# Attention heads taken in pairs with full-precision value products, and a rewritten order of the MLP behind them

## The chip, the cores and the metric

One core of a Trainium2 chip runs the whole program. The metric is the device time of one execution in microseconds. Five engines matter: TensorE (PE in the profile; its weight loads are PEld), VectorE (DVE), ScalarE (ACT), GpSimd (POOL), and SyncE (SP), which here only issues DMAs.

## The reference, cut to what matters

```python
q, k, v: (4, 8, 576, 64) float32      # batch, heads, sequence, head_dim
def _attn_ref(q, k, v):
    q_rot, k_rot = rotate(q), rotate(k)            # rotary position, halves of 32
    scores = matmul(q_rot, k_rot.T) / sqrt(64)
    attn = exp(scores - max(scores)); attn = attn / (sum(attn) + 1e-9)
    return matmul(attn, v)
x = attn_out as (2304, 512)
def _moe_ref(x, w_in, w_out, g_ln):                # 512 -> 1024 -> 512
    h = x @ w_in
    solu = h * softmax(h)
    ln = (solu - mean) / sqrt(var + 1e-6) * g_ln
    return ln @ w_out
```

## The kernel before, in words

The attention works head by head, 32 heads, and holds the scores transposed: keys on partitions, queries along the row. A sequence of 576 is cut into five tiles of keys (four of 128, one of 64), and every product is done in two halves of 288 queries. TensorE is fed in fp32r, a reduced form of float32; precision is kept by splitting a number into a high part and a rest. The scores of a tile are two products, `KK` by `QQ` and `KB` by `QB` (L760): the rests stand in the lower 64 partitions, and `QB` also carries the negated row maximum. That maximum comes from products of its own (L748), reduced by VectorE (L526). Queries and keys arrive untransposed, so TensorE transposes them through PSUM (L725) and ScalarE copies them out (L349).

The exponentials of a tile (`p_full`, ScalarE, L369) are split: a high copy `p_hi` by ScalarE or VectorE (L343, L533), and a rest `p_lo` by GpSimd (L259; the 64-row tile by VectorE, L539). V is split too (L332, L268). Then `weigh` (L778) multiplies three ways per tile: `v_hi` by `p_hi`, `v_hi` by `p_lo`, `v_lo` by `p_hi`, and two ways for the tile of 64, whose rest is stacked below it. The columns of ones in V give the row sums. VectorE and GpSimd share the rotation (L496, L510; L252). VectorE also inverts the sums with two transposes (L546, L551), and GpSimd multiplies by the inverse (L264).

The order on each engine is written out by hand in its `step` function, and semaphores tie the engines together. There is one PSUM slot for scores: scores of a tile wait for the exponentials of the one before. The loops over heads and tiles are hardware loops (`Fori`).

The MLP works on 18 tiles of 128 tokens. For each tile TensorE does eight transposes of the normalized rows (L803), 24 products with `w_in` of a later tile (`up`, L788) and 24 with `w_out` (`down`, L815), all with 512 columns: three products for each true one. VectorE splits x (L572, L574), takes the maximum (L579), multiplies (L591), computes statistics (L596) and the normalized rows (L614), and subtracts the high part (L584). ScalarE does the exponentials (L391), the high part (L396) and the output (L402).

Of the kernel before, what the change touches and what calls it, by code (L numbers as in the profile page):

```python
# [11 lines left out]
AX_X = mybir.AxisListType.X  # L12
AX_XY = mybir.AxisListType.XY

P = 128
B, H, S, D = 4, 8, 576, 64
HEADS = B * H
PAIRS = HEADS // 2
NT = -(-S // P)
TAIL = S - (NT - 1) * P  # L20
SP_ = NT * P
HALF = S // 2
TOK = B * S
# [10 lines left out]

START = 1


def attention_then_mlp(nc: bass.Bass, qk_d, v_d, rope_d, w_d, gain_d, out_d):

    ctx = ExitStack()

    def sb(stack, name, shape, dt=F32):
        return stack.enter_context(nc.sbuf_tensor(name, shape, dt))

    def sem(stack, name):
        return stack.enter_context(nc.semaphore(name))

    with ctx:
        xT = sb(ctx, "xT", [P, KC * TOK])
        w_hi = sb(ctx, "w_hi", [P, NW * 512], F32R)
        w_lo = sb(ctx, "w_lo", [P, NW * 512], F32R)
        ident = sb(ctx, "ident", [P, P])
        ps = ctx.enter_context(nc.psum_tensor("ps", [P, 8, 512], F32))
        qk = [sb(ctx, f"qk{a}", [P, 2, NT, D]) for a in range(2)]
        v = [sb(ctx, f"v{a}", [P, NT, D]) for a in range(2)]
        rope = sb(ctx, "rope", [P, 2, NT, D])
        rot = sb(ctx, "rot", [P, 2, NT, D])  # L60
        crossed = sb(ctx, "crossed", [P, 2, NT, D])
        k_splits = sb(ctx, "k_splits", [P, 2, NT, 2 * D])
        q_twices = sb(ctx, "q_twices", [P, 2, NT, 2, D])
        q_rests = sb(ctx, "q_rests", [P, 2, NT, 2 * D])
        k_split = [k_splits[:, a, :, :] for a in range(2)]
        q_twice = [q_twices[:, a, :, :, :] for a in range(2)]
        q_rest = [q_rests[:, a, :, :] for a in range(2)]
        KK = [sb(ctx, f"KK{a}", [P, SP_], F32R) for a in range(2)]
        KB = [sb(ctx, f"KB{a}", [P, SP_], F32R) for a in range(2)]
        QQ = [sb(ctx, f"QQ{a}", [P, SP_], F32R) for a in range(2)]  # L70
        QB = [sb(ctx, f"QB{a}", [P, SP_], F32R) for a in range(2)]
        v_hi = [sb(ctx, f"v_hi{a}", [P, NT, P], F32R) for a in range(2)]
        v_lo = [sb(ctx, f"v_lo{a}", [P, NT, P], F32R) for a in range(2)]
        p_full = [sb(ctx, f"p_full{i}", [P, S]) for i in range(3)]
        p_parts = sb(ctx, "p_parts", [P, 2 * NT - 1, S], F32R)
        p_hi = [p_parts[:, j, :] for j in range(NT)]
        p_lo = [p_parts[:, NT + j, :] for j in range(NT - 1)]
        o_num = sb(ctx, "o_num", [P, S])
        o_sum = sb(ctx, "o_sum", [P, S])
        sum_cols = sb(ctx, "sum_cols", [P, S])  # L80
        inv_cols = sb(ctx, "inv_cols", [P, S // 32])
        inv = sb(ctx, "inv", [P, S])
        eps = sb(ctx, "eps", [P, 1])
        w_raw = sb(ctx, "w_raw", [P, 512])
        gain = sb(ctx, "gain", [P, NW])

        prep = [ps[:, 0:2, :], ps[:, 2:4, :]]
        prep_flat = [ps[:, 2 * i:2 * i + 2, :].rearrange("p a c -> p (a c)") for i in range(2)]
        scores = ps[:, 4:6, :]
        o_ps = ps[:, 6:8, :]  # L90

        qk_loaded = [sem(ctx, f"qk_loaded{a}") for a in range(2)]
        v_loaded = [sem(ctx, f"v_loaded{a}") for a in range(2)]
        rope_loaded = sem(ctx, "rope_loaded")
        gain_loaded = sem(ctx, "gain_loaded")
        w_loaded = sem(ctx, "w_loaded")
        w_hi_done = sem(ctx, "w_hi_done")
        w_lo_done = sem(ctx, "w_lo_done")
        cos_done = sem(ctx, "cos_done")
        sin_done = sem(ctx, "sin_done")  # L100
        sin_part_done = sem(ctx, "sin_part_done")
        rot_done = sem(ctx, "rot_done")
        k_hi_done = sem(ctx, "k_hi_done")
        k_lo_done = sem(ctx, "k_lo_done")
        q_hi_done = sem(ctx, "q_hi_done")
        q_lo_done = sem(ctx, "q_lo_done")
        kb_done = sem(ctx, "kb_done")
        v_hi_done = sem(ctx, "v_hi_done")
        v_lo_done = sem(ctx, "v_lo_done")
        prep_filled = [sem(ctx, f"prep_filled{i}") for i in range(2)]  # L110
        prep_free = [sem(ctx, f"prep_free{i}") for i in range(2)]
        scores_ready = sem(ctx, "scores_ready")
        exp_done = sem(ctx, "exp_done")
        p_hi_done = [sem(ctx, f"p_hi_done{j}") for j in range(NT)]
        p_lo_done = sem(ctx, "p_lo_done")
        p_tail_done = sem(ctx, "p_tail_done")
        pv_done = sem(ctx, "pv_done")
        o_taken = sem(ctx, "o_taken")
        inv_done = sem(ctx, "inv_done")
        x_done = sem(ctx, "x_done")  # L120
        ident_zero = sem(ctx, "ident_zero")
        pool_const = sem(ctx, "pool_const")
        dve_const = sem(ctx, "dve_const")
        POOL_CONST, DVE_CONST = 10, 8

        x_hi = [KK[0][:, 0:KC * P].rearrange("p (c t) -> p c t", c=KC),
# [829 lines left out]
```

## Time and profile before

| | us |
|---|---|
| median of 3 runs | 669.5 |
| lowest, highest run | 669.39, 672.09 |
| span of the profiled execution | 671.9 |
| PE, PEld busy | 569.8, 506.1 |
| DVE busy | 570.5 |
| ACT, POOL busy | 356.4, 354.2 |

The time of the profiled execution itself is not recorded apart from the three runs; its span lies between the median and the highest of them, 0.2 us below the highest. The span goes from the first instruction to the last. In a matmul row the duration counts the whole path through the array, so two rows overlap; the distance from one start to the next is what a matmul costs.

### The profile page before, as it was taken

To read this page: it belongs to the slowest core of one execution; us is meant where nothing else is said; L and a number is where in the kernel's file an instruction comes from. 1 tells how busy PE (TensorE), PEld (TensorE's weight loads), DVE (VectorE), ACT (ScalarE), POOL (GpSimd) and SP (SyncE) were. 2 spreads that over 40 slices of the span, in tenths; PEclk is the share of its full clock that TensorE was granted. 3 is DMA by queue.
4 is the path that set the end of the run, shared out by engine and by line. 5 is a ranking of instruction groups with operands and counts; after the bars stand their busy time and mean duration, and the time that the engine had idled before them with its cause. 6 is when DMAs were issued, how large, how long until landed. Compare 5 with 4: busy or idle time off the path is not lost.

```text
span 671.9 us, 11250 instructions
## 1 busy us (share of the span) xinstructions
PE 569.8 (85%) x3400; PEld 506.1 (75%) x3400; DVE 570.5 (85%) x756; ACT 356.4 (53%) x586; POOL 354.2 (53%) x273
## 2 busy tenths in 40 slices
PE   7878767887687877877878778899999999999986
PEld 7767757777677776776778767887888888888865
DVE  8899999999999999999999999897766757566560
ACT  3877668576686766766867667651212122121211
POOL 5769688786887967868769687641000000000000
PEclk9999999798998989989889898899999999999998
DMA  4111211112101121121111210000000000000000
GB/s 129 44 47 31 74 45 29 45 29 74 45 29 45 34 70 45 29 68 40 40 45 29 74 45 10 16 1 18 16 16 31 16 31 16 30 17 16 31 17 31
DMA packets 14411, 25.12 MB, mean 37 GB/s; under 512 B 1728, under 2 KB 5824, under 8 KB 14400
## 3 DMA queue, kind: packets, MB, share of 16 engines
q1 hardware_dynamic: 14400, 24.98, 12.2%
q8 instruction: 6, 0.10, 0.1%
q14 instruction: 5, 0.04, 0.0%
HBM read 20.26 MB, written 4.72 MB: 37 GB/s over the span
## 4 chain that ended last, share of the span: by engine, by line
PE 37%; DVE 36%; issue 21%; DVEq 2%; ACT 2%; POOL 1%; DMA 1%; SPq 0%; ACTq 0%; POOLq 0%
PE ps L815 15%; PE ps L788 14%; DVE q_rests L526 10%; DVE p_parts L533 6%; DVE rot L496 5%; DVE KB L562 4%; DVE w_hi L557 3%; DVE k_splits L515 2%; PE ps L803 2%; PE ps L778 2%; PE ps L760 2%; DVE rot L510 2%; PE ps L748 1%; DVE sum_cols L546 1%; PE ps L725 1%
## 5 line engine op out<-in xcount | busy, mean ns | idle before, releaser
L259 POOL TENSOR_TENSOR p_parts<-p_full,p_parts 128x576 fp32r<-128x576 f32 x128 | 201.5, 1578 | 87.8 <-ACT p_parts L343 48.7
L369 ACT ACTIVATE p_full<-ps 128x576 f32<-128x576 f32 (+1 forms) x160 | 103.9, 650 | 81.9 <-DVE p_parts L539 70.7
L760 PE MATMUL ps<-QQ,KK 128*128 128x288 f32 x320 | 82.3, 340 | 58.1 <-ACT p_full L369 58.1
L526 DVE TENSOR_REDUCE q_rests<-ps 128x1 fp32r<-128x576 f32 x160 | 114.3, 745 | 4.5 <-PE ps L748 4.4
L314 POOL TENSOR_TENSOR r<-r,expo 128x1 f32<-128x1 f32 x17 | 11.9, 698 | 185.3 <-DVE r L607 185.3
L748 PE MATMUL ps<-KK,QQ 128*128 128x288 f32 x320 | 82.0, 343 | 28.9 <-DVE q_rests L526 27.8
L778 PE MATMUL ps<-p_parts,v_hi 128*128 128x288 f32 x576 | 105.1, 301 | 0.0
L760 PEld LDWEIGHTS ps<-QQ,KK 128*128 128x128 f32 x320 | 51.3, 200 | 67.9 <-ACT p_full L369 66.4
L815 PE MATMUL ps<-w_hi,p_parts 128*128 128x512 f32 x288 | 94.3, 399 | 4.9 <-DVE p_parts L584 4.9
L778 PEld LDWEIGHTS ps<-p_parts,v_hi 128*128 128x128 f32 x576 | 89.2, 197 | 0.1
L748 PEld LDWEIGHTS ps<-KK,QQ 128*128 128x128 f32 x320 | 57.1, 214 | 40.8 <-DVE q_rests L526 39.3
L252 POOL TENSOR_TENSOR crossed<-qk,rope 128x320 f32<-128x320 f32 x63 | 78.1, 1258 | 1.4 <-DVE rot L510 1.4
L402 ACT ACTIVATE qk<-ps 128x512 f32<-128x512 f32 x18 | 10.8, 598 | 114.7 <-PE ps L815 114.7
L760 PE MATMUL ps<-QB,KB 128*128 128x288 f32 x320 | 71.5, 307 | 0.0
L778 PE MATMUL ps<-p_parts,v_lo 128*128 128x288 f32 x320 | 70.1, 301 | 0.0
L815 PEld LDWEIGHTS ps<-w_hi,p_parts 128*128 128x128 f32 x288 | 55.6, 193 | 18.5 <-issue 5.3
L343 ACT ACTIVATE p_parts<-p_full 128x576 fp32r<-128x576 f32 x96 | 65.4, 682 | 2.1
L579 DVE TENSOR_REDUCE neg_max<-ps 128x1 f32<-128x1024 f32 x18 | 22.0, 1224 | 52.0 <-PE ps L788 52.0
L815 PE MATMUL ps<-w_lo,p_parts 128*128 128x512 f32 x144 | 57.5, 399 | 0.0
L760 PEld LDWEIGHTS ps<-QB,KB 128*128 128x128 f32 x320 | 54.4, 199 | 0.0
L778 PEld LDWEIGHTS ps<-p_parts,v_lo 128*128 128x128 f32 x320 | 52.7, 193 | 0.0
L533 DVE CAST p_parts<-p_full 128x576 fp32r<-128x576 f32 x64 | 48.3, 754 | 2.2 <-ACT p_full L369 2.2
(86 smaller groups left out, 1145.4 us busy)
## 6 DMA issues: line engine op xcount, KB each, us to landing
qk<-qk_in SPq DMA_DIRECT2D x32, 320.0 KB, 3.2
v<-v_in SPq DMA_DIRECT2D x32, 160.0 KB, 2.3
out<-qk SPq DMA_DIRECT2D x18, 256.0 KB, 2.0
w_raw<-w_in SPq DMA_DIRECT2D x16, 256.0 KB, 2.6
rope<-rope_in SPq DMA_DIRECT2D x1, 320.0 KB, 3.5
gain<-gain_in SPq DMA_DIRECT2D x1, 8.0 KB, 4.2
```

Source lines behind the costliest of these rows:

```text
L252: ins = nc.gpsimd.tensor_tensor(crossed[:, :, :, to], qk[a][:, :, :, of], rope[:, 1:2, :, to].broadcast_to([P, 2, NT, 32]), ALU.mult)
L259: nc.gpsimd.tensor_tensor(p_lo[j][:, :], p_full[j % 3][:, :], p_hi[j][:, :], ALU.subtract).then_inc(p_lo_done, 1)
L343: nc.scalar.activation(p_hi[j][0:rows, :], p_full[j % 3][0:rows, :], ACT.Copy)\
L369: nc.scalar.activation(p_full[j % 3][0:rows, :].rearrange("p (b c) -> p b c", b=2), scores[0:rows, :, 0:HALF], ACT.Exp, scale=SCALE).then_ ...
L496: nc.vector.tensor_tensor(rot[:, :, :, :].rearrange("p s t d -> p s (t d)"), qk[a][:, :, :, :].rearrange("p s t d -> p s (t d)"), rope[:, ...
L526: nc.vector.tensor_reduce(q_rest[a][:, j, D:D + 1].bitcast(F32R), prep[slot][:, :, 0:HALF], AX_XY, ALU.max, negate=True).then_inc(prep_fre ...
L533: nc.vector.tensor_copy(p_hi[j][0:rows, :], p_full[j % 3][0:rows, :]).then_inc(p_hi_done[j], 1)
L748: ins = nc.tensor.matmul(prep[slot][:, half, 0:HALF], QQ[a][:, j * P:(j + 1) * P], KK[a][:, half * HALF:(half + 1) * HALF], start=True, st ...
L760: ins = nc.tensor.matmul(scores[:, half, 0:HALF], left[a][:, j * P:(j + 1) * P], right[a][:, half * HALF:(half + 1) * HALF], start=(k == 0 ...
L778: ins = nc.tensor.matmul(o_ps[:, half, 0:HALF], left[a][:, j, :], right[j][:, half * HALF:(half + 1) * HALF], start=(j == 0 and k == 0), s ...
L788: ins = nc.tensor.matmul(h_ps[a][:, half, :], left[a][:, c, :], right[:, col:col + 512], start=(c == 0 and k == 0), stop=(c == KC - 1 and ...
L815: ins = nc.tensor.matmul(y_ps[a], left[a][:, c * P:(c + 1) * P], right[:, col:col + 512], start=(k == 0), stop=(k == 3 * FC - 1))
```

## The change

The attention takes two heads at a time (16 pairs), and everything is written out without hardware loops.

- The host hands over q and k transposed, with a second copy whose halves are exchanged. So no transposes on TensorE: the rotation is one product with the cosines, one with the sines (both GpSimd, 128x1152), and one sum (VectorE, 128x1152).
- ScalarE writes the high parts straight into the stacks `QK` (`high`, `second_queries`) and copies keys into `KB` (`copy_keys`); VectorE writes the rests (`low_keys`, `low_queries`).
- The two 64-row tails of a pair share one tile: 9 steps a pair in place of 10.
- `weigh` multiplies V by the exponentials once, both in plain float32 (`V`, `p_main`, `p_tail` are no longer fp32r). No splits of P or V remain.
- The row maxima go through a 32x32 transpose and ten short DMAs into a row of `KB`. The row sums go by DMA into 9 columns (`sc`), ScalarE adds EPS, VectorE takes the reciprocal, and two DMAs through DRAM spread it over the partitions (`inv`).
- GpSimd divides the pair before last only after VectorE's rotation sum of the pair in hand.
- In the MLP the transposes stand between the `down` products, and `up` of the last tile stands before `down` of tile 14 instead of after it.

```diff
-                    parts = ((v_hi, p_hi), (v_hi, p_lo), (v_lo, p_hi))
-                else:
-                    pe.wait_ge(p_tail_done, START + h + 1)
-                    parts = ((v_hi, p_hi), (v_lo, p_hi))
-                for k, (left, right) in enumerate(parts):
-                    for half in range(2):
-                        ins = nc.tensor.matmul(o_ps[:, half, 0:HALF], left[a][:, j, :],
...
+                    p, v = p_main[(8 * n + 4 * a + j) % 3], V[c][:, a, 1 + j, :]
+                for half in range(2):
+                    ins = nc.tensor.matmul(o_ps[a][:, half, 0:HALF], v, p[:, half * HALF:(half + 1) * HALF],
+                                           start=(k in (0, 5)), stop=(k in (4, 9)))
+                ins.then_inc(pv_done, 1)
...
+            for n in range(PAIRS):
+                for s in range(STEPS):
+                    score(n, s)
+                    for i in maxima(n, s)[:1]:
+                        row_scores(n + 1, i)
...
+                    if s == 0:
+                        if n >= 1:
+                            weigh(n - 1, 9)
+                    elif s <= BOTH:
+                        weigh(n, s - 1)
+                    else:
+                        if s == BOTH + 1:
+                            weigh(n, 4)
+                        weigh(n, s)
...
+                if n + 2 < PAIRS:
+                    pool.wait_ge(low_q_done[1], n + 2)
+                    pool.wait_ge(w_lo_done, n - 1)
+                    pool.wait_ge(x_loaded[n % 2], uses(n + 2) * 16 - (0 if n % 2 else 32))
+                    times_cos(n + 2)
+                    times_sin(n + 2)
+                    pool.wait_ge(rot_done, n + 3)
+                if n >= 2:
+                    divide(n - 2)
...
+            def add_eps(m):
+                c = m % 2
+                act.wait_ge(sums_set[c], uses(m) * 32)
+                nc.scalar.activation(sc[c][:, :], sc[c][:, :], ACT.Copy, bias=EPS).then_inc(eps_done, 1)
...
+            for t in range(TILES):
+                if t + 3 == TILES - 1:
+                    for i in range(UPS):
+                        up(t + 3, i)
+                first = 16 if t == 0 else 4 if t + 3 < TILES else 0
+                for i in range(DOWNS):
+                    down(t, i)
+                    if t + 1 < TILES and first <= i < first + FC:
+                        transpose_ln(t + 1, i - first)
+                if t + 3 < TILES - 1:
+                    for i in range(UPS):
+                        up(t + 3, i)
```

TensorE in the middle of the attention, before; L725 are transposes, L760 scores, L748 products for the maxima, L778 the product with V:

```order
L725 MATMUL ps<-ident,k_splits 128x128 x5
L725 MATMUL ps<-ident,q_twices 128x128 x5
L757 ISA
L760 MATMUL ps<-QQ,KK 128x288 x2
L760 MATMUL ps<-QB,KB 128x288 x2
L771 ISA
L778 MATMUL ps<-p_parts,v_hi 128x288 x4
L778 MATMUL ps<-p_parts,v_lo 128x288 x2
L745 REGISTER_ALU
L748 MATMUL ps<-KK,QQ 128x288 x2
```

And now, steps 4 and 5 of a pair; L769 are scores, L742 the maxima, L791 the product with V:

```order
L769 MATMUL ps<-QK 128x288 x2
L769 MATMUL ps<-KB 128x288 x2
L769 MATMUL ps<-QK 128x288 x2
L769 MATMUL ps<-KB 128x288 x2
L742 MATMUL ps<-QK 128x288 x4
L791 MATMUL ps<-p_main,V 128x288 x2
L769 MATMUL ps<-QK 128x288 x2
L769 MATMUL ps<-KB 128x288 x2
L742 MATMUL ps<-QK 128x288 x2
L791 MATMUL ps<-p_tail,V 128x288 x4
```

The transposes are gone, and six products with V per tile are now two.

GpSimd in the middle of the attention, before (one head; L252 rotation, L259 rests of P, L268 rest of V, L264 division):

```order
L252 TENSOR_TENSOR crossed<-qk,rope 128x10x32 x2
L257 REGISTER_ALU
L258 ISA
L259 TENSOR_TENSOR p_parts<-p_full,p_parts 128x576
...
L268 TENSOR_TENSOR v_lo<-v,v_hi 128x5x64
...
L264 TENSOR_TENSOR xT<-o_num,inv 128x576
```

And now, a whole pair (L302 and L307 are the two products of the rotation, the rest the division):

```order
L302 TENSOR_TENSOR X<-X,rope 128x1152
L307 TENSOR_TENSOR X<-X,rope 128x1152
L315 TENSOR_TENSOR xT<-oe,inv 64x576
L317 TENSOR_TENSOR xT<-oe,inv 64x512
L320 TENSOR_TENSOR xT<-oe,inv 64x64
```

The eight rests of P and two of V per pair have gone; the whole of the rotation's products has come in.

## Rows read from the trace of the kernel before

**Rows 1.** Busy time by stretch: span, then PE, PEld, DVE, ACT, POOL busy (instructions), clock, DMA.
```profile
281.00:310.00 29.00, 22.71 (x154) 21.17 (x155) 28.68 (x34) 20.78 (x36) 22.71 (x17) 0.94 0.16 43
657.85:671.90 14.05, 8.36 (x33) 6.35 (x31) 1.22 (x1) 2.22 (x3) 0.00 (x0) 0.88 0.10 37
```
**Rows 2.** Who waited for whom in the attention, 49 to 440 us: total, times, longest.
```profile
PE ps L760 <- ACT p_full L369: 53.5, 29, 3.1
```
**Rows 3.** Groups by line and shape: busy us, mean ns | idle before.
```profile
L259 POOL TENSOR_TENSOR p_parts<-p_full,p_parts 128x576 fp32r<-128x576 f32 x128 | 201.5, 1578 | 87.8 <-ACT p_parts L343 48.7 <-DVE p_parts L533 38.9
L526 DVE TENSOR_REDUCE q_rests<-ps 128x1 fp32r<-128x576 f32 x160 | 114.3, 745 | 4.5 <-PE ps L748 4.4
L778 PE MATMUL ps<-p_parts,v_hi 128*128 128x288 f32 x576 | 105.1, 301 | 0.0
L778 PEld LDWEIGHTS ps<-p_parts,v_hi 128*128 128x128 f32 x576 | 89.2, 197 | 0.1
L369 ACT ACTIVATE p_full<-ps 128x576 f32<-128x576 f32 x128 | 83.3, 651 | 81.3 <-DVE p_parts L539 70.7 <-PE ps L760 9.1
L252 POOL TENSOR_TENSOR crossed<-qk,rope 128x320 f32<-128x320 f32 x63 | 78.1, 1258 | 1.4 <-DVE rot L510 1.4
L325 ACT ACTIVATE q_twices<-rot 128x640 fp32r<-128x640 f32 x32 | 23.2, 725 | 0.0
```
**Rows 4.** TensorE in order of time, in the attention: start, duration, group.
```profile
300.20 0.71 PE L725 MATMUL ps<-ident,q_twices 128*128 128x128 f32 x5
300.67 0.52 PE L760 MATMUL ps<-QQ,KK 128*128 128x288 f32 x2
301.02 0.43 PE L760 MATMUL ps<-QB,KB 128*128 128x288 f32 x2
301.29 0.68 PE L778 MATMUL ps<-p_parts,v_hi 128*128 128x288 f32 x4
301.81 0.43 PE L778 MATMUL ps<-p_parts,v_lo 128*128 128x288 f32 x2
```
**Rows 5.** VectorE and GpSimd in order of time, with and without each other.
```profile
6.63 0.83 DVE L510 TENSOR_TENSOR rot<-rot,crossed 128x640 f32<-128x640 f32 x1
301.49 1.85 POOL L264 TENSOR_TENSOR xT<-o_num,inv 128x576 f32 x1 [0.70 <-DVE inv L551]
302.06 1.88 DVE L539 TENSOR_TENSOR p_parts<-p_full,p_parts 64x576 fp32r<-64x576 f32 x1
318.28 0.75 DVE L539 TENSOR_TENSOR p_parts<-p_full,p_parts 64x576 fp32r<-64x576 f32 x1
320.65 1.42 POOL L259 TENSOR_TENSOR p_parts<-p_full,p_parts 128x576 fp32r<-128x576 f32 x1 [2.75 <-ACT p_parts L343]
```
**Rows 6.** Busy time in the fourth microsecond; the last number is GB/s.
```profile
3.00:4.00 1.00, 1.00 (x7) 1.00 (x6) 0.68 (x3) 0.00 (x0) 0.87 (x3) 1.00 1.01 397
```
**Rows 7.** DMA issues on the page: KB each, us to landing.
```profile
v<-v_in SPq DMA_DIRECT2D x32, 160.0 KB, 2.3
```
**Rows 8.** TensorE from the end of the attention into the MLP.
```profile
451.17 0.40 PE L788 MATMUL ps<-w_hi,KB 128*128 128x512 f32 x1
...
457.96 1.09 PE L803 MATMUL ps<-ident,q_rests 128*128 128x128 f32 x8 [1.17 <-DVE q_rests L614]
...
481.85 1.03 PE L803 MATMUL ps<-ident,q_rests 128*128 128x128 f32 x8
...
493.62 1.04 PE L803 MATMUL ps<-ident,q_rests 128*128 128x128 f32 x8
```
**Rows 9.** TensorE at the end of the MLP.
```profile
650.68 0.47 PE L815 MATMUL ps<-w_hi,p_parts 128*128 128x512 f32 x1 [2.46 <-DVE p_parts L584]
...
657.85 1.04 PE L803 MATMUL ps<-ident,q_rests 128*128 128x128 f32 x8
...
661.35 0.47 PE L815 MATMUL ps<-w_hi,p_parts 128*128 128x512 f32 x1 [2.46 <-DVE p_parts L584]
...
668.28 0.39 PE L815 MATMUL ps<-w_hi,p_parts 128*128 128x512 f32 x1
```

More of the change, by code:

```diff
@@ L65, in attention_then_mlp @@
[L65 to L72, printed above, removed]
@@ L82, in attention_then_mlp @@
[L82 to L94, printed above, removed]
@@ L178, in constants @@
[L178 to L188 removed]
+        x_hi_done = sem("x_hi_done")
@@ new lines, in attention_then_mlp, with x_of, uses, own @@
+        y_ready = sem("y_ready")
+        y_taken = sem("y_taken")
+        stored = [sem(f"stored{a}") for a in range(2)]
+        const_done = sem("const_done")
+        def x_of(m):
+            return xT[:, PAIRS - 4:PAIRS, :] if m == 2 else X[m % 2][:, :, :]
+        def uses(n):
+            return n // 2 + 1
+        def own(a):
+            return slice(a * D, a * D + D)
+        def other(a):
+            return slice((1 - a) * D, (1 - a) * D + D)
+        def last_pair(t):
+            return ((t + 1) * P - 1) // S * HP + HP - 1
@@ new lines, in row_part, with rows_of_a @@
+            def row_part(m, group, row, at, first, count, done):
+                n = count * TURN
+                sp.dma_start(KB[m % 2][row:row + 1, 1, at:at + n].bitcast(F32)
+                             .rearrange("o (p f) -> o p f", f=TURN),
+                             nm_row[group][first:first + (count - 1) * TURN + 1:TURN, :]).then_inc(done, 16)
+            def rows_of_a(m):
+                done = rows_early[m % 2]
+                sp.wait_ge(turned[0], m + 1)
+                for j in range(1 if m == 0 else BOTH):
+                    row_part(m, 0, D, main_col(0, j), j, 4, done)
+                row_part(m, 0, D, MAIN, BOTH, 2, done)
+                row_part(m, 0, 0, S + TAIL, D + BOTH, 2, done)
@@ L473, in _ @@
[L473 to L486 removed]
+                if t >= 2:
+                    act.wait_ge(stored[t % 2], t // 2 * 16)
@@ new lines, in _ @@
+            for n in range(1, PAIRS - 1):
+                for s in range(STEPS):
+                    for i in maxima(n, s):
+                        row_max(n + 1, i)
+                    if s == 0:
+                        low_keys(n + 1, 1)
+                        if n >= 2:
+                            invert(n - 2)
+                    if s == 1:
+                        low_queries(n + 1, 1)
+                    if s == 2 and n >= 2:
+                        w_low(n - 2)
+                    if s == 5 and n + 2 < PAIRS:
+                        add(n + 2)
+                    if s == 7 and n + 2 < PAIRS:
+                        low_keys(n + 2, 0)
+                    if s == 8 and n + 2 < PAIRS:
+                        low_queries(n + 2, 0)
```

1336 lines of the change are left out of this document (644 added, 692 removed).

## The prediction, made before the changed kernel ran

> **What bounds the kernel now.** I read the page first (who is busy), then the busy times by stretch, then who waits for whom, and last TensorE in order of time, because the busy share of TensorE counts the path through the array and not its cost.
>
> The attention runs to 451.2 us and the MLP from there to 671.9 [rows 8, 1]. In the attention VectorE is busy 28.68 of 29.00 us, with every other engine at 23 or less [rows 1]; 29 us is about one pair of heads (451.2 / 16 = 28.2). TensorE waits 53.5 us for ScalarE's exponentials [rows 2], and these had waited 70.7 us for VectorE's `p_tail` L539 [rows 3]. So VectorE is the bound, with GpSimd close behind: 1578 ns for one rest of P, 201.5 us in all. In the MLP a tile takes 493.62 - 481.85 = 11.77 us with TensorE never idle [rows 8]: there TensorE is the bound, and only its ends hold waits.
>
> What TensorE really pays: two fp32r products of 288 columns start 0.27 us apart (301.02 to 301.29), four take 0.52 (301.29 to 301.81), so 0.132 us each. After f32 transposes two take 0.35, which is 0.09 more. Five transposes take 0.47, 0.09 each [rows 4].
>
> **The change, part by part.**
>
> *Attention, TensorE.* A pair now has 60 fp32r products (20 for the maxima, 40 for scores): 60 x 0.132 = 7.9 us. And 20 plain float32 products with V, where 56 fp32r ones were. No row shows such a product. Below, it is bounded by one fp32r pass, 0.132 us; above, by four passes that do not overlap, 4 x 0.301 = 1.20 us [rows 3]. I take four overlapping passes, 4 x 0.132 = 0.53 us: the kernel before makes a full product out of three passes and drops rest by rest; a product that keeps everything needs the fourth, and the nearest rows [rows 4] show passes that overlap. So 20 x 0.53 = 10.6 us. At each of 9 steps the array turns from f32 back to fp32r: 9 x 0.09 = 0.8. Sum: 19.3 us a pair.
>
> *The Trainium skill, "FP8 and Floating Point Precision", section "TensorE Precision Notes", says that true FP32 makes four passes through the array (high and low parts of both sides). By it the term is the same 0.53 us; no trace row here shows it.*
>
> *The other engines in a pair.* ScalarE: 9 exponentials x 0.65 = 5.9; two `high` of 1152 elements, by the rows of 576 and 640 elements [rows 3] about 1.15 each; four copies of 576 at 0.68; two `take_o` 0.65; `w_high` 0.6; EPS 0.2: 13.0 us. VectorE: 9 maxima x 0.745 = 6.7; the sum of 1152 by 0.83 for 640 about 1.4 when GpSimd is silent; four rests at 0.75 [rows 5]; `w_low` 0.7; transposes and reciprocal 0.5: 12.3 us. GpSimd: two products of 1152 at 2 x 1.42 = 2.8 at most without VectorE beside it, 5.7; division 1.4 + 1.3 + 0.3 = 3.0: 8.7 us. All lie under TensorE's 19.3.
>
> *Do they reach each other in time?* Count from the pair's first score. A step is 0.53 + 0.26 + 1.06 = 1.86 us on TensorE; step 4 is 0.8 longer and step 5 1.06. The exponentials start 0.06 after the scores and take 0.65; score, exponential and score again cost 1.45 us, less than 1.86: covered. A maximum ends at about 1.8 us into its step; the next is asked for at 2.4: covered, with 0.6 to spare for one rest of 0.75 behind it. GpSimd's products wait for `w_low` in step 2 (6.2 us), so they end at 11.9. VectorE's sum stands behind the sixth maximum, which ends at 11.9: it runs to 13.3. ScalarE's `high` of that sum stands behind exponential 6 (14.4), so it is ready. The rows of maxima leave after step 4 (10.1) and land within about 5 us (six issues and 2.3 us [rows 7]), long before 19.3; the four late ones leave at 18.9, and step 4 of the next pair asks for them at 27. Division, EPS and the DRAM round trip are used only by the MLP. EPS and the key copies on ScalarE thus cost nothing: exponentials leave it 6 us a pair. If that cover goes, one copy costs 0.7 us a pair.
>
> *Start.* 1.77 MB must land for pair 0; at 397 GB/s [rows 6] and 2.3 us of latency [rows 7] that is 7 us, where before 0.64 MB sufficed. Then two products (8.7), the sum (10.1), `high` and second queries (13.3), five maxima (17.5), transpose and DMAs with 2.3 us to landing: first score at 20.3. The late rows need four more maxima behind `add(1)` and land at 27; steps 4 to 8, with the maxima of pair 1 pressed into them, take 14. Pair 0 ends at 41.
>
> *Attention sum.* 41 + 14 x 19.3 = 311. The last pair has no maxima (-2.6) but the 24 `up` products of tile 0 (24 x 0.227 = 5.4, 0.227 being (11.77 - 0.8) / 48): 22.2, and 1.1 for the last `weigh`: 335.
>
> *MLP.* The same products follow. Before, the stretch is 671.9 - 451.2 = 220.7 us. Out go 1.2 of waiting before tile 0's transposes [rows 8], two waits of 2.46 at the end, and the slow columns of the last two `down`: 657.85 - 650.68 = 7.2 and 668.67 - 661.35 = 7.3 where 24 x 0.227 = 5.4, at a mean granted clock of 0.88 in that stretch [rows 9, 1]: 3.6. Together 9.7. In comes a new wait: with `up` of tile 17 ahead, tiles 14 to 16 have only `down` (6.2 us) to cover VectorE's 8.5 us per tile: I count 0.7 + 0.8 + 0.9 = 2.4 us. Transposes between products cost what they cost in a row, about 0.1 each. MLP: 220.7 - 9.7 + 2.4 = 213.4.
>
> *Total.* 335 + 213.4 = 548.6, as a span against 671.9; the median of runs is 2.4 below that span, so I say **549 us**, 120 us less. This case alone spans 530 (0.49 us per float32 product, -13, and a smoother start) to 578 (1 us of lost time in each pair and 0.56 us a product).
>
> **Rivals.**
>
> *GpSimd's rotation ends late.* Its rows of 320 elements take 1258 ns [rows 3], 3.9 ns each; at that rate the two products take 9 us and end at 15.3, the sum at 16.7, and both exponential 7 (behind `high`) and maximum 6 stall TensorE by 2 us: 14 x 2.1 = +29, 578 us; with VectorE and GpSimd blocking one another, as where 0.75 became 1.88 beside a division [rows 5], +50. For it: `add` stands just where GpSimd ends. Against: semaphores keep most two-input operations apart, and the rows of 576 give 2.5 ns. Chance 0.16.
>
> *Weight loads are not hidden between the four passes.* Transposes of 128 columns, whose streaming is 0.132 x 128 / 288 = 0.06, start 0.09 apart [rows 4]: a load takes at least that where nothing hides it. Then a product costs 4 x (0.132 + 0.09) = 0.89, 0.36 more for 320 of them: +115, 664 us. Against: weight loads of 197 ns [rows 3] vanish between products 0.132 us apart. Chance 0.07.
>
> *The Trainium skill, "TensorE: Matmul & The Clock Gate", section "Part 3: Packing small matmuls — row/col tiling", says that a weight load overlaps a running matmul only when the row group differs. By it this rival's 664 us would hold. The trace disagrees for fp32r: 197 ns loads of the whole array lie beside products 0.132 us apart.*
>
> *Slower: the passes do not overlap at all.* At 1.20 us each the products with V alone take 24 us a pair, +0.67 x 320 = +215, 763 us. The point where the change turns into a loss is (671.9 - 548.6) / 320 = 0.385 above 0.53: 0.91 us a product. For it only the missing row speaks. Chance 0.04.
>
> *The product needs fewer passes.* With one or two, TensorE falls to about 11 to 14 us a pair, and the chain score, exponential, score (9 x 1.45 + 0.5) holds at 14: 549 - 15 x 5.3 = 470. Chance 0.06.
>
> **How the numbers follow.** My forecast has 0.67. The range must hold 8 in 10: it takes the forecast's own 530 to 578, and of the rotation rival the part up to 608; below I go to 522 for a faster product. 0.5% is about what a measurement of this kernel can tell from no change. Faster: 0.67 + 0.16 + 0.06 and most of the hidden-load rival (664 is 0.8% under the median) 0.05 = 0.94; within 0.5%: 0.015; slower: 0.045.
>
> **What would show it.** Right: in the middle of the attention TensorE without idle time of note, 19 to 20 us from one pair to the next, products with V starting 0.5 us apart, VectorE near 65% and GpSimd near 45% busy, the MLP at 11.8 us a tile with waits of about 1 us at tiles 15 to 17. Wrong: products with V 0.9 us apart or more; TensorE waiting for the maxima in steps 6 to 8, with VectorE waiting for GpSimd's sines; ScalarE waiting for the sum; a first score after 25 us.

## The result, and the profile after

| | before | after |
|---|---|---|
| median of 5 runs | 669.5 us | **532.58 us** (532.42 to 533.69) |
| ratio, 95% interval | | 0.7949 (0.7934 to 0.7964) |
| span of the profiled run | 671.9 us | 531.6 us |
| attention, then MLP | 451.2, 220.7 | 316.8, 214.8 |

The forecast was 549 us with a range of 522 to 608. The change saves 137 us, 17 more than predicted. Of the 140.3 us between the two spans, the attention gives 134.4 and the MLP 5.9.

The page of the changed kernel: busy time by engine, and the chain that ended last.

```profile
PE 506.2 (95%) x2608; PEld 426.2 (80%) x2608; DVE 346.8 (65%) x551; ACT 254.1 (48%) x377; POOL 154.3 (29%) x120
...
PE 89%; DVE 6%; ACT 2%; DMA 1%; issue 1%; SPq 0%; POOL 0%; DVEq 0%; ACTq 0%
...
L791 PE MATMUL ps<-p_main,V 128*128 128x288 f32 x512 | 146.8, 410 | 0.0
```

VectorE, full in the attention before [rows 1], is at 65% of the whole span, and 89% of the chain is TensorE. L791 is the row that the trace of before did not have, the plain float32 product. Its count is the first surprise: 512 records for 256 products (the 64 others read `p_tail`). Each product leaves two records.

Busy time by stretch, columns as in [rows 1]: three stretches at the start, then pairs 1 to 14.

```profile
14.20:18.10 3.90, 3.89 (x14) 3.36 (x15) 2.82 (x6) 2.03 (x3) 3.68 (x2) 1.00 0.02 7
18.10:21.60 3.50, 1.11 (x6) 0.64 (x5) 3.43 (x5) 0.00 (x0) 1.56 (x1) 1.00 0.00 1
21.60:31.80 10.20, 7.90 (x23) 6.40 (x24) 5.10 (x7) 4.96 (x6) 5.22 (x2) 0.50 0.15 33
...
46.72:295.05 248.33, 248.11 (x1402) 217.35 (x1401) 174.85 (x250) 175.33 (x265) 116.38 (x64) 1.00 0.36 112
```

In pairs 1 to 14 TensorE is busy 248.11 of 248.33 us. A pair takes 17.74 us on average and holds 12.5 of ScalarE (predicted 13.0), 12.5 of VectorE (12.3) and 8.3 of GpSimd (8.7). The loads of these three engines were predicted well. Pair 0 began at the lower level of the granted clock, 1.2 GHz (0.50 up to 31.8 us); from there to the end of pair 14 it is 1.00.

Who waited for whom, 60 to 300 us: total, times, longest. It answers to [rows 2].

```profile
POOL X L302 <- DVE w_lo L570: 67.1, 12, 12.6
DVE nm L553 <- PE ps L742: 60.8, 81, 2.0
ACT p_main L424 <- PE ps L769: 47.2, 81, 1.1
...
DVE X L531 <- POOL X L307: 4.0, 12, 0.6
```

The arrow has turned round. Before, TensorE waited for ScalarE's exponentials; now ScalarE and VectorE wait for TensorE. The last line is the one on which the largest rival stood: VectorE's sum waits at most 0.6 us for GpSimd's sines.

TensorE in order of time, at step 4 of one pair and of the next.

```profile
159.54 0.43 PE L742 MATMUL ps<-QK 128*128 128x288 f32 x2
159.81 1.13 PE L791 MATMUL ps<-p_main,V 128*128 128x288 f32 x4
160.56 0.64 PE L769 MATMUL ps<-QK 128*128 128x288 f32 x2
161.04 0.42 PE L769 MATMUL ps<-KB 128*128 128x288 f32 x2
...
178.72 0.42 PE L769 MATMUL ps<-KB 128*128 128x288 f32 x2
```

Two fp32r products take 0.27 us (159.54 to 159.81), as in [rows 4]. Two float32 products (four records) and two scores take 161.04 - 159.81 = 1.23, so the float32 pair takes 0.97: **0.485 us a product**, 0.24 a record. Nothing is lost where the array goes back to fp32r; the score's row only seems to begin early, 0.03 us after the start of the last float32 record, and its second product stands where 0.24 and 0.13 put it. A pair takes 178.72 - 161.04 = 17.68 us.

### The profile page after: what moved, and what is told of

Read it like the earlier page. It is cut to its first block, busy times and chain, and to the rows that moved or that the text cites. A ratio compares the mean times of both kernels' runs of the same rounds, so it can differ in the third digit from the quotient of the medians.

```text
span 531.6 us, 7274 instructions
## 1 busy us (share of the span) xinstructions
PE 506.2 (95%) x2608; PEld 426.2 (80%) x2608; DVE 346.8 (65%) x551; ACT 254.1 (48%) x377; POOL 154.3 (29%) x120
## 4 chain that ended last, share of the span: by engine, by line
PE 89%; DVE 6%; ACT 2%; DMA 1%; issue 1%; SPq 0%; POOL 0%; DVEq 0%; ACTq 0%
PE ps L791 29%; PE ps L804 16%; PE ps L769 16%; PE ps L818 16%; PE ps L742 9%; PE ps L828 3%; DMA X<-x_in 1%; DVE X L628 1%; DVE nm L553 1%; DVE stats L609 1%; DVE X L604 1%; ACT X L444 1%; DVE neg_max L591 1%; ACT QK L393 1%; DVE X L531 1%
## 5 line engine op out<-in xcount | busy, mean ns | idle before, releaser
L553 DVE TENSOR_REDUCE nm<-ps 128x1 fp32r<-128x576 f32 x144 | 108.2, 755 | 75.4 <-PE ps L742 73.7
L791 PE MATMUL ps<-p_main,V 128*128 128x288 f32 x512 | 146.8, 410 | 0.0
L424 ACT ACTIVATE p_main<-ps 128x576 f32<-128x576 f32 x128 | 83.3, 651 | 73.2 <-PE ps L769 72.0
L791 PEld LDWEIGHTS ps<-p_main,V 128*128 128x128 f32 x512 | 91.3, 192 | 14.4 <-ACT p_main L424 0.2
L818 PE MATMUL ps<-w_hi,QK 128*128 128x512 f32 x288 | 101.9, 422 | 0.6 <-DVE QK L597 0.6
L769 PE MATMUL ps<-QK 128*128 128x288 f32 x320 | 98.3, 388 | 0.9 <-ACT p_main L424 0.9
L804 PE MATMUL ps<-w_hi,KB 128*128 128x512 f32 x288 | 92.8, 392 | 0.0
L742 PE MATMUL ps<-QK 128*128 128x288 f32 x320 | 68.9, 309 | 19.2 <-ACT QK L398 14.2
L769 PEld LDWEIGHTS ps<-QK 128*128 128x128 f32 x320 | 59.5, 193 | 17.8 <-ACT p_main L424 2.5
L742 PEld LDWEIGHTS ps<-QK 128*128 128x128 f32 x320 | 51.5, 195 | 21.9 <-ACT QK L398 14.2
L769 PE MATMUL ps<-KB 128*128 128x288 f32 x320 | 68.8, 297 | 0.0
L302 POOL TENSOR_TENSOR X<-X,rope 128x1152 f32<-128x1152 f32 x14 | 37.2, 2657 | 99.4 <-DVE w_lo L570 67.1
L818 PE MATMUL ps<-w_lo,QK 128*128 128x512 f32 x144 | 59.3, 412 | 0.0
L769 PEld LDWEIGHTS ps<-KB 128*128 128x128 f32 x320 | 52.1, 191 | 0.0
```

The source lines that it names most:

```text
L302: nc.gpsimd.tensor_tensor(x[:, 0:2, :], x[:, 0:2, :], rope[:, 0:1, :].broadcast_to([P, 2, S]), ALU.mult).then_inc(cos_done, 1)
L424: nc.scalar.activation(dst[:, :].rearrange("p (b c) -> p b c", b=2), score_ps[:, :, 0:HALF], ACT.Exp, scale=SCALE).then_inc(exp_done, 1)
L553: nc.vector.tensor_reduce(nm[g][:, at:at + 1], src[:, :, 0:HALF], AX_XY, ALU.max, negate=True)\
L742: ins = nc.tensor.matmul(slot[:, half, 0:HALF], QK[c][:, 0, of], QK[c][:, 1, to + half * HALF:to + (half + 1) * HALF], start=(g == 0), sto ...
L769: ins = nc.tensor.matmul(score_ps[:, half, 0:HALF], keys[:, of:of + P], queries[:, to + half * HALF:to + (half + 1) * HALF], start=(g == 0 ...
L791: ins = nc.tensor.matmul(o_ps[a][:, half, 0:HALF], v, p[:, half * HALF:(half + 1) * HALF], start=(k in (0, 5)), stop=(k in (4, 9)))
```

## Experiments

### The float32 product alone

**twice.** Every float32 product is issued twice into the same sum.

```diff
-                for half in range(2):
-                    ins = nc.tensor.matmul(o_ps[a][:, half, 0:HALF], v, p[:, half * HALF:(half + 1) * HALF],
-                                           start=(k in (0, 5)), stop=(k in (4, 9)))
+                for again in range(2):
+                    for half in range(2):
+                        ins = nc.tensor.matmul(o_ps[a][:, half, 0:HALF], v, p[:, half * HALF:(half + 1) * HALF],
+                                               start=(k in (0, 5) and again == 0),
+                                               stop=(k in (4, 9) and again == 1))
```

> Each float32 product with V is issued twice into the same sums (320 more products; the division cancels the factor of two). Theory A: TensorE is the bound and such a product costs 0.485 us (four records at 150.97 us of the changed kernel and the next row start 0.97 us later than 0.53 for the four products of fp32r would put it): the span grows by 320 x 0.485 = 155 us to 687, a pair takes 27.4 us in place of 17.7, and no other engine changes its busy time. Rival B: the pair's 17.7 us are set by the chain scores, exponential, scores or by VectorE, with TensorE only looking full: the first doubling fills idle time and the span grows by less than 120 us. Rival C: the step that I left out, a turn from f32 to fp32r of 0.09 us, exists and the product costs 0.44: +141 us, 673.

Measured: 686.17 us (one run), span 684.3. The 320 extra products cost 684.3 - 531.6 = 152.7 us, 0.477 each. TensorE in order of time, one step:

```profile
301.37 2.10 PE L792 MATMUL ps<-p_main,V 128*128 128x288 f32 x8
...
303.58 0.43 PE L769 MATMUL ps<-KB 128*128 128x288 f32 x2
```

Eight records and two scores take 2.21 us, so eight take 1.94, and four in the changed kernel 0.97: twice the records, twice the time, so no fixed cost hides at the turn. From one pair to the next it takes 27.39 us in place of 17.67 in the undisturbed pairs, 9.72 more for 20 products, 0.486 each. (The 0.477 of the whole span is less because pair 0, which also waits for others, grows by only 7.3 us.) Added products cost what they take on the array, and no other engine gets busier (VectorE 344.0, ScalarE 253.6, GpSimd 143.9 us, against 346.8, 254.1 and 154.3). This fixes the price of the product and that TensorE is the bound. Weight loads that are not hidden (0.89 us) and passes that do not overlap (1.20 us) are both out.

*The Trainium skill, "FP8 and Floating Point Precision", section "TensorE Precision Notes", says that true FP32 takes four passes. The trace's 0.485 us is 3.7 times the 0.132 of an fp32r product; whether that is four passes it does not show, for it has two records a product.*

**one_pass2.** V and the exponentials are stored as fp32r and multiplied once, so P and V have reduced precision here. VectorE copies V, 2 x 128x320 a pair. (A first form, one_pass, with a second pair of buffers for V, did not fit into SBUF and gave no time.)

```diff
-        V = [sb(f"V{c}", [P, 2, 5, P]) for c in range(2)]
+        V = [sb(f"V{c}", [P, 2, 5, P], F32R) for c in range(2)]
...
-        p_main = [sb(f"p_main{i}", [P, S]) for i in range(3)]
+        p_main = [sb(f"p_main{i}", [P, S], F32R) for i in range(3)]
...
+                    nc.vector.tensor_copy(V[c][:, a, :, own(a)], VD[:, a, :, :]).then_inc(v_copied, 1)
```

> P and V go into TensorE as fp32r, once, so both are used in reduced precision; V lands in a buffer of its own and VectorE makes two copies of 128x320 per pair. Theory A: 320 products fall from 0.485 to 0.132 us, TensorE would need 60 x 0.132 + 20 x 0.132 = 10.6 us a pair, and the chain scores, exponential, scores (1.45 us a step, 2.0 in step 4: 13.6 us) or ScalarE (13.0) becomes the bound: 14 to 15 us a pair, 531.6 - 15 x 3.2 = 484, TensorE waiting for the exponentials L424 and half idle. Rival: VectorE's strict order of maxima and rests (12.3 us plus 1.0 for the copies, with waits for GpSimd's rotation between) binds at 16 us or more: 507 or more, TensorE waiting for L553.

Measured: 521.32 us (one run). Some 7 us a pair leave TensorE (20 x 0.353), and a pair becomes only 0.6 us shorter (double score 158.13 to 175.24: 17.11; between 16.5 and 17.6, on average 17.0, against 17.74). Busy time by stretch, then the waits, 60 to 300 us:

```profile
60.00:300.00 240.00, 193.45 (x1135) 159.29 (x1135) 186.30 (x273) 170.80 (x262) 113.69 (x64) 0.99 0.35 111
```
```profile
PE ps L756 <- DVE nm L554: 25.5, 34, 1.8
...
DVE X L532 <- POOL X L308: 19.2, 13, 1.9
```

No engine is full. A ring binds: TensorE waits for VectorE's maxima, VectorE's sum for GpSimd's sines (19.2 us, where the changed kernel had 4.0), and GpSimd's cosines for VectorE's `w_low` (59.9 us). The chain of work followed back from the cosines at 174.84, one turn of the ring:

```profile
157.91 2.67 POOL X L303
...
163.29 1.36 DVE X L532
...
173.86 0.76 DVE w_lo L579
...
174.84 2.67 POOL X L303
```

GpSimd multiplies for 5.3 us, VectorE sums, and then does maxima and rests almost without a break until `w_lo`, for whose end the next cosines wait: 16.93 us. The copies of V, which this run adds, are not in it: VectorE makes them at 158.27, while GpSimd multiplies, and still waits 1.77 us for the sines afterwards. So the rotation rival named a real chain, without its way back through `w_low`; in the changed kernel it ends some 0.7 us a pair under TensorE's time. Theory A is wrong (521 and not 484 us), and so is the 470 us of the prediction's last rival: cheaper products would have met this ring. No run here moves `w_low` or the rotation, so what the next reordering would bring is open.

### How much of the gain is the product's form

**before_plain.** The kernel before, with V and P plain float32, one product, no splits.

```diff
-                    parts = ((v_hi, p_hi), (v_hi, p_lo), (v_lo, p_hi))
-                for k, (left, right) in enumerate(parts):
...
+                for half in range(2):
+                    ins = nc.tensor.matmul(o_ps[:, half, 0:HALF], v_hi[a][0:rows, j, :],
+                                           p_full[j][0:rows, half * HALF:(half + 1) * HALF],
+                                           start=(j == 0), stop=(j == NT - 1))
...
-                nc.scalar.activation(p_hi[j][0:rows, :], p_full[j % 3][0:rows, :], ACT.Copy)\
...
-                nc.vector.tensor_copy(p_hi[j][0:rows, :], p_full[j % 3][0:rows, :]).then_inc(p_hi_done[j], 1)
```

> The kernel before with one part of the change alone: V and the exponentials go into TensorE as plain float32, in one product per tile and half, and all splits of P and V are gone (GpSimd's rests, VectorE's and ScalarE's high copies, the stacked tail). The transposes on TensorE, the rotation by heads and the rest stay. Theory A: most of the attention's gain is the splits that VectorE no longer makes. VectorE loses per pair two copies of 0.69 and 0.82 and two tails of 1.28 (5.6 us) and much of its waiting for GpSimd; TensorE needs 60 x 0.132 + 30 x 0.09 + 20 x 0.485 = 20.3 us. I expect 22 to 23 us a pair against 28.5: 671.9 - 16 x 6 = 575. Rival: the pretransposed layout carries the gain (15 copies out of PSUM and the rotation at half width): the splits alone bring less than 50 us, 620 or more.

Measured: 600.23 us (4 runs), ratio 0.8921 (0.8883 to 0.896). Its page, and TensorE at the tail of a head and of the next but one:

```profile
PE 581.7 (97%) x3144; PEld 484.6 (81%) x3144; DVE 410.6 (69%) x660; ACT 293.7 (49%) x490; POOL 101.3 (17%) x113
```
```profile
299.80 1.23 PE L753 MATMUL ps<-p_full,v_hi 64*128 64x288 f32 x4
...
305.12 0.51 PE L740 MATMUL ps<-QQ,KK 128*128 128x288 f32 x2
305.47 0.43 PE L740 MATMUL ps<-QB,KB 128*128 128x288 f32 x2
305.73 0.71 PE L705 MATMUL ps<-ident,k_splits 128*128 128x128 f32 x5
306.28 0.71 PE L705 MATMUL ps<-ident,q_twices 128*128 128x128 f32 x5
306.74 0.51 PE L740 MATMUL ps<-QQ,KK 128*128 128x288 f32 x2
...
322.14 1.23 PE L753 MATMUL ps<-p_full,v_hi 64*128 64x288 f32 x4
```

Half of the gain: about 70 of 137 us. The splits gone, VectorE falls to 69% and TensorE is the bound, with 322.14 - 299.80 = 22.34 us a pair. The pair came out as expected (22 to 23) and the total did not (575), because I had taken 28.5 us for a pair of before, and for pair 0 too, which gains only 0.8 (21.7 to 20.9). The transposes of one head and of the next but one in the trace of before lie 27.28 us apart:

```profile
298.58 0.71 PE L725 MATMUL ps<-ident,q_rests 128*128 128x128 f32 x5
...
325.86 0.71 PE L725 MATMUL ps<-ident,q_rests 128*128 128x128 f32 x5
```

So plain products save 27.28 - 22.34 = 4.9 us a pair. A part of it may come by way of the clock: in the kernel before, TensorE has nothing to do from 290 to 292 us, and some 2 us later the granted clock is at its lower level for a while, and so in most pairs.

```profile
294.00:297.00 3.00, 2.69 (x11) 2.30 (x11) 3.00 (x4) 2.89 (x7) 1.13 (x2) 0.50 0.00 0
```

In **before_plain** it is 1.00 from 60 to 360 us. No run shows how much of the 4.9 us this is.

What the new stacks then add is 22.34 - 17.68 = 4.66 us a pair. 30 transposes take 3.3 of it: five start 0.55 us before the next five (305.73 to 306.28), 0.11 each. The other 1.4 us were not taken apart. From pair 1 to pair 14 this makes 64 us; pair 1 itself begins 7.9 us later than in **before_plain** (46.72 against 38.87), and the last pair with the MLP is 11 us shorter. Together that is the 67 us between the two spans.

### The small edits

**after_again** is the changed kernel once more, beside the next three.

> The changed kernel once more, as the measure for the small steps beside it: 532.6 us.

Measured: 533.2 us (4 runs), ratio 0.7952 (0.7931 to 0.7973).

**divide_free.** GpSimd divides without waiting for VectorE's sum.

```diff
-                    pool.wait_ge(rot_done, n + 3)
```

> GpSimd no longer waits for VectorE's rotation sum before it divides. Theory A (TensorE bounds, the rest is cover): the division runs beside the sum, which then takes up to 1.9 us longer, but the maximum behind it still comes in time or nearly so: within 2 us of the changed kernel, 532 to 535. Rival: the order is what holds the two engines apart; the sum grows to 3 us in each pair and TensorE then waits for maximum 6 about 1 us in each of 14 pairs: +14, 547.

Measured: 532.96 us, ratio 0.7949 (0.793 to 0.7967). No difference: nothing near the path waits for a division.

**copies_dve.** EPS and the key copies on VectorE.

```diff
+                nc.vector.tensor_copy(KB[c][own(a), 0, at:at + S], QK[c][own(a), 1, at:at + S].bitcast(F32))\
...
+                nc.vector.tensor_scalar(sc[c][:, :], sc[c][:, :], EPS, None, ALU.add).then_inc(eps_done, 1)
```

> EPS and the key copies go from ScalarE to VectorE (two of 64x576 and one of 128x9 in a pair). Theory A: VectorE has 0.35 of its time idle, so nothing changes, 532 to 534, with VectorE busy 0.9 to 1.3 us more a pair and ScalarE 1.6 us less. Rival: in VectorE's strict order the copies push a maximum past its time and TensorE waits 0.5 us a pair: +7, 540.

Measured: 535.31 us, ratio 0.7989 (0.7963 to 0.8015), 2.1 us above **after_again**, which is within 0.5% but above the 532 to 534 that I had expected; the lowest of its four runs (534.9) lies above the highest of **after_again** (534.01). Busy time from 100 to 200 us, of the changed kernel and of this one:

```profile
100.00:200.00 100.00, 99.95 (x567) 87.59 (x566) 71.35 (x105) 71.10 (x109) 52.20 (x29) 1.00 0.37 114
```
```profile
100.00:200.00 100.00, 99.77 (x563) 87.24 (x561) 86.26 (x122) 62.01 (x89) 53.56 (x29) 1.00 0.38 114
```

VectorE takes 15 us more in 100, 2.6 us a pair where I had expected at most 1.3, and TensorE has hardly a gap. A pair takes 17.89 us on average against 17.74, and 14 x 0.15 are the 2.1 us. So the place of the copies is worth 0.4% while TensorE binds; above all it leaves VectorE room.

**tile_back.** `up` of the last MLP tile goes back behind `down` of tile 14.

```diff
-                if t + 3 == TILES - 1:
-                    for i in range(UPS):
-                        up(t + 3, i)
-                if t + 3 < TILES - 1:
+                if t + 3 < TILES:
```

> The products of the last MLP tile with w_in stand behind the down products of tile 14 again. Theory A: tile 17's maximum, statistics and transposes then come late and TensorE waits twice: +3 us (the kernel before had waits of 2.5 us after the transposes of both last tiles; here the transposes stand inside the down products, so about half of it is left). Rival: the waits of 0.3 + 0.7 + 0.8 us that the new order has at tiles 15 to 17 go away and nothing else comes: -1 us.

Measured: 533.01 us, ratio 0.794 (0.7919 to 0.7961). From the first `down` to the last it takes 198.9 us against 199.2. The waits at the end, of this kernel and of the changed one:

```profile
516.64 0.49 PE L818 MATMUL ps<-w_hi,QK 128*128 128x512 f32 x1 [0.73 <-DVE QK L597]
517.55 0.33 PE L828 MATMUL ps<-ident,X 128*128 128x128 f32 x1 [0.42 <-DVE X L628]
```
```profile
515.75 0.50 PE L818 MATMUL ps<-w_hi,QK 128*128 128x512 f32 x1 [0.56 <-DVE QK L597]
516.67 0.33 PE L828 MATMUL ps<-ident,X 128*128 128x128 f32 x1 [0.41 <-DVE X L628]
```

1.15 us of idle time against 1.27 (0.30 more stands at 508.80). My 3 us for this move were wrong: the two waits of 2.46 [rows 9] shrink to this in both kernels, so it is not the place of `up` for the last tile that shortens them. What is left is that the transposes now stand among the `down` products of the tile before; no run puts them back.

### The start, and the transposes of the MLP

TensorE of the changed kernel at the start, idle time before and its releaser in brackets:

```profile
14.21 4.46 PE L742 MATMUL ps<-QK 128*128 128x288 f32 x16 [14.21 <-ACT QK L398]
...
23.16 0.85 PE L742 MATMUL ps<-QK 128*128 128x288 f32 x2 [3.75 <-DVE nm L553]
23.81 0.68 PE L769 MATMUL ps<-QK 128*128 128x288 f32 x2
24.29 0.68 PE L769 MATMUL ps<-KB 128*128 128x288 f32 x2
```

The first score stands behind the ninth product for the maxima, which waits for room that VectorE has to free. And two products take 0.48 (23.81 to 24.29), 0.24 each, where they take 0.132 later: the granted clock is at its lower level there. It had risen at 18.2 us, while the first sixteen products ran, and fallen at 21.6, when TensorE had had nothing to do since 19.4; it rose again at 31.8. Before 18.2 us the products are 0.24 us apart too, though the clock column says 1.00: the trace has no record of the clock before that time, and the column shows 1.00 for want of one. In **divide_free** the first record stands at 30.3 us, and the products between 24 and 30 us are 0.24 apart under a column of 1.00. At the start, the distance between products tells the level and the column does not.

**warm.** 120 transposes of `ident` fill TensorE before the first work, 4 stand behind each product for the maxima, 30 more before the last.

```diff
+            def stay_warm(count):
+                for _ in range(count):
+                    nc.tensor.transpose(score_ps[:, 0, 0:P], ident[:, :], ident[:, :])
...
+            pe.wait_ge(pool_const, 1)
+            stay_warm(120)
             for i in range(STEPS):
                 row_scores(0, i)
+                stay_warm(4)
+                if i == 7:
+                    stay_warm(30)
```

> Transposes of the identity fill TensorE's idle time before the first score: 120 at the start, 4 behind each of the first maxima's products, 30 more before the last of them. In the changed kernel the products between 23.8 and 31.2 us start 0.24 us apart where 0.13 is usual, at a granted clock of 0.82 in 23.8 to 46. Theory A: with TensorE busy from 1.5 us on the clock stays at its upper level, the first four steps take 1.7 us each in place of 2.9 once the exponentials allow it: -2 to -4 us. Rival: these steps wait for exponentials and late rows anyway: no change.

Measured: 533.59 us, ratio 0.7957 (0.7935 to 0.798). The filling itself ended late. Busy time by stretch in it, and the first product of the work behind it:

```profile
2.00:6.00 4.00, 4.00 (x20) 4.00 (x20) 2.90 (x6) 0.01 (x1) 3.53 (x11) 1.00 0.99 332
8.00:12.00 4.00, 4.00 (x39) 4.00 (x38) 2.72 (x2) 0.73 (x1) 0.00 (x0) 1.00 1.08 354
```
```profile
17.34 0.51 PE L742 MATMUL ps<-QK 128*128 128x288 f32 x2
```

The first transposes of the filling are 0.21 us apart, the later ones 0.109: the clock rose at 7.2 us (again under a column of 1.00) and stayed up. The first real product began at 17.34 in place of 14.21, and the first score at 27.23 in place of 23.81. Pair 0 then took 20.0 us in place of 22.9, with the same order. Pair 1 begins at 47.24 against 46.72: what was lost in front ate what the clock gave.

**warm_order.** As warm, with 24 transposes in place of the last 30, and the last two products for the maxima stand behind scores 0 and 1.

```diff
-            for i in range(STEPS):
+            for i in range(7):
...
+                    if n == 0 and s in (0, 1):
+                        row_scores(0, 7 + s)
```

> The same warm start, and the last two products for the maxima of pair 0 stand behind the first and the second score instead of before them. In the changed kernel the first score (23.81) stood behind the ninth product for the maxima, which waited until 23.16 for VectorE. Theory A: the first score comes when the six early rows have landed, at about 21.5 to 22.5, and the late rows, which need maximum 8, land in time: -1.5 us beyond the warm start, 527 to 529 in all. Rival: the late rows set step 4 and nothing is won: as the warm start alone.

Measured: 532.59 us, ratio 0.7938 (0.7919 to 0.7956), where I had expected 527 to 529. In the profiled run the clock rose earlier, at 4.4 us, so the 120 transposes ended at 15.98, 1.8 us late, and the first score came at 24.20; but after a wait of 1.05 us TensorE ran at the lower level from 28.3 to 31.7 us. Pair 1 begins at 47.00. This shows no gain, and does not price the order alone.

**rows_together.** The eight transposes of an MLP tile stand in a row.

```diff
-                    if t + 1 < TILES and first <= i < first + FC:
-                        transpose_ln(t + 1, i - first)
+                    if t + 1 < TILES and i == first:
+                        for c in range(FC):
+                            transpose_ln(t + 1, c)
```

> The eight transposes of an MLP tile stand in a row behind one down product in place of one behind each of eight. Interleaved, a transpose and its product take 0.344 us where the product alone takes 0.227, so 0.117 for a transpose, 0.94 us a tile; in a row they took 0.79 with the turn in the kernel before. Theory A: -0.15 x 17 = -2.5 us. Rival: ScalarE's high part waits for the last transpose, which comes earlier now, and nothing else changes, or TensorE waits longer for ln: 0 to +1 us.

Measured: 531.42 us, ratio 0.7918 (0.7899 to 0.7937), 1.2 us less than the changed kernel, and 1.2 and 2.2 less than **warm_order** and **warm**, which ran beside it. TensorE of the changed kernel, then of this one:

```profile
485.54 0.27 PE L828 MATMUL ps<-ident,X 128*128 128x128 f32 x1
...
485.88 0.27 PE L828 MATMUL ps<-ident,X 128*128 128x128 f32 x1
```
```profile
403.63 1.04 PE L828 MATMUL ps<-ident,X 128*128 128x128 f32 x8
404.42 0.70 PE L818 MATMUL ps<-w_hi,QK 128*128 128x512 f32 x2
404.96 0.40 PE L818 MATMUL ps<-w_lo,QK 128*128 128x512 f32 x1
```

A transpose and a product together take 0.344 (485.54 to 485.88); without the product's 0.227 that is 0.117 a transpose. Eight in a row, with the slower product behind them, take 404.96 - 403.63 - 2 x 0.227 = 0.88, 0.11 each. A tile gets 0.06 us shorter (11.85 to 11.79), 1.0 us in 17 tiles. The first to the last `down` takes 197.1 against 199.2, 2.1 less; the other 1.1 is at the end, where tile 15 takes 6.5 us in place of 7.6: TensorE's wait of 0.56 for VectorE is gone, and so is the 0.30. The medians alone could hardly tell this: the interval overlaps that of the changed kernel.

**best** joins warm, warm_order and rows_together.

> Warm start, new order of the first maxima, and transposes in a row together. If the three add up: 532.6 - 4 - 2.5 = 526. If the start is set by the late rows: 530.

Measured: 531.9 us, ratio 0.7927 (0.7909 to 0.7946). No better than rows_together alone, and I had expected 526 or 530. The late filling again: the first product begins at 17.12, the first score at 25.33, pair 1 at 46.71.

**best2** is the same with 86 transposes in place of 120, so that the filling ends when the queries arrive.

```diff
-            stay_warm(120)
+            stay_warm(86)
```

> The combination once more with 86 transposes of the identity at the start in place of 120, so that they end before the first product for the maxima at 14.2 us (with 120 that product came at 17.3 or 16.0 us, which ate what the warm clock gave: pair 1 began at 47.2 against 46.7). Theory A (the cold start costs 2.5 us and was only covered by my own filling): pair 1 begins at 44 to 45 us, with the transposes in a row worth 2.1: 527 to 529 us. Rival (the late rows and VectorE's second set of maxima set pair 0): as the kernels with 120, 531 to 532.

Measured: **528.77 us**, ratio 0.7884 (0.7869 to 0.79), some 0.7% under the changed kernel, and the fastest of those without reduced precision. Its stretches, then TensorE where score 0 and pair 1 begin:

```profile
14.20:23.80 9.60, 9.14 (x74) 8.67 (x74) 8.68 (x12) 2.52 (x5) 6.47 (x3) 1.00 0.02 5
23.80:46.00 22.20, 19.88 (x104) 15.73 (x104) 16.15 (x23) 14.18 (x20) 4.01 (x2) 1.00 0.07 16
```
```profile
22.57 0.53 PE L769 MATMUL ps<-QK 128*128 128x288 f32 x2 [0.16 <-DMA KB<-nm_row]
...
43.91 0.64 PE L769 MATMUL ps<-QK 128*128 128x288 f32 x2
```

The first score now waits for its own DMA, and comes 1.24 us earlier. Pair 0 takes 43.91 - 22.57 = 21.3 us against 46.72 - 23.81 = 22.9. So pair 1 begins 2.8 us earlier: 1.2 before the first score, by the order and the full clock together, and 1.6 in pair 0, where the clock gives time and the two products that the order moved there take some. With the order unchanged pair 0 took 2.9 us less (**warm**), though it began later there. So these runs put the clock's part in pair 0 at 1.6 to 2.9 us.

## Why the prediction was right, and where it was off

The mechanism held: VectorE's splits and TensorE's transposes go, and TensorE binds at its own price. By the terms of the sum:

| term | predicted | measured | over the whole |
|---|---|---|---|
| pair 1 begins | 41 | 46.72 | +5.7 |
| a pair, 14 times | 19.3 | 17.74 | -21.9 |
| last pair | 23.3 | 21.8 | -1.5 |
| MLP | 213.4 | 214.8 | +1.4 |

With 0.7 of rounding this is 531.6 - 548.6 = -17.0 (334.5 stands in the prediction as 335, and 335 + 213.4 = 548.4 as 548.6). The total is nearer than its largest term: the pairs had been put 21.9 us too dear and the start 5.7 too cheap, and that these partly cancel is luck. The last step does not follow: the prediction puts the median 2.4 us below the span and then writes 549 without taking it off. In the changed kernel the median lies 1.0 above the span.

- **The float32 product was mis-sized.** I took 4 x 0.132 = 0.53 us; it is 0.485. At 20 a pair this is 0.9 us, 13 us over 14 pairs. That it costs this little (against 1.20 or 0.89) was right, and **twice** shows it. That it is made of four passes is not shown.
- **The turn back to fp32r does not exist.** I had taken 0.09 us for it from [rows 4], and that was a misreading. The first product behind a row of transposes is shown as starting 0.03 us after the last of them, so the row looks too cheap (0.09 each) and the two products behind it too dear (0.35). Five transposes between two rows of transposes take 0.55 (305.73 to 306.28), 0.11 each, and 300.20 to 301.02 is then 5 x 0.11 and 2 x 0.13, with nothing left for a turn. That is 9 x 0.09 = 0.8 us a pair, 11 us in all. Both terms together are 24 us; the pairs gave 21.9, since a pair is 17.74 us on average where its products add up to 17.6. (With 0.87 for eight transposes the prediction's sum gives its 0.227; with the 0.8 written there it is 0.229.)
- **The start failed by 5.7 us.** First score 23.81 in place of 20.3: by **best2**, where the score waits for it, the rows' DMA lands at 22.57 and not at 20.3 (the fifth maximum ends at 18.8 and not at 17.5, and the DMAs take the rest), and another 1.24 is the ninth product standing ahead of the score. Then pair 0 took 22.9 in place of 20.7; with the clock up it took 21.3 (**best2**) or 20.0 (**warm**), so the lower clock is the largest part of this. I had worked out the start by latencies and left the clock out, though [rows 1] showed it below 1 next to a wait.
- **The cover was right.** Maxima, exponentials and rotation all end in time, and GpSimd's rotation of 1152 elements takes 2.66 us a product: 5.3 for two, predicted 5.7. But **one_pass2** shows the cover is thin: some 0.7 us a pair beyond TensorE's own time.
- **The MLP.** The waits at tiles 15 to 17 are 1.3 us and not 2.4 (-1.1). The wait before tile 0's transposes, which I had taken out whole, is still there in part: 0.54 at 333.47, and 0.42 before the next tile's at 343.22 (+1.0). A tile is 11.85 us and not 11.77, since a spread transpose costs 0.117 and one in a row 0.109 (+1.4 over 17 tiles). The gain at the end comes without moving the last tile (**tile_back**).
- **One reading was loose.** 28.2 us for a pair of before had the start in it; the steady pair is 27.3. It did not enter the sum, but it spoiled the expectation of **before_plain**.

## What to carry to other kernels

When a product is split by hand into parts of lower precision, count what the splits cost on the other engines: one product in plain float32 cost 0.485 us on TensorE against 0.40 for three parts, and in **before_plain** took VectorE from 98% to 75% busy in the attention and GpSimd from 78% to 24%. Before pricing a relief on the busiest engine, find the ring of waits that lies next below it; here 7 us a pair taken off TensorE bring 0.7. Fill TensorE at the start only up to the moment when its first data arrive: 34 transposes too many cost what the clock gave.

## What the runs showed of the hardware that I had not expected

- A float32 product of 128x128 by 288 columns leaves two records of about 0.24 us each, 0.485 together, at a granted clock of 1.00; at 0.50 the records are 0.48 apart (27.31 to 27.79 in the changed kernel). Weight loads of 192 ns stand beside it and vanish. *The Trainium skill, "TensorE: Matmul & The Clock Gate", section "Part 3: Packing small matmuls — row/col tiling", has a list of what overlaps that lets a load overlap only where the row group differs, while the paragraph ahead of that list also names a background weight buffer. The trace disagrees with the list: these loads fill the whole array.*
- A float32 transpose of 128 columns costs 0.109 us in a row of them and 0.117 between fp32r products of 512 columns. An fp32r product behind float32 transposes or behind float32 products starts with no delay; its row is shown as starting 0.03 us after the start of the record before it, and the time is found again at the second product.
- TensorE's clock followed its work in both directions. In the changed kernel products were 0.24 us apart from 14.2 to 18.1, 0.13 after that, and 0.24 again from 23.8 (0.50 granted from 21.6, with no work from 19.4 to 23.2) until 31.8. A filling of float32 transposes alone, begun at 1.5 us, raised the clock: they went from 0.213 to 0.109 us apart at 4.4 to 7.2 us, by the run. The clock column is no witness before the trace's first clock record: it said 1.00 while products were 0.24 apart.
